# A linear-attention and mixture kernel on one core: receptances and state as fp16 pairs, and the low part of the values on GpSimd

## The reference

```python
# stage 1, for 4 batches and 8 heads, 768 tokens, 48 dims a head
for t in range(S):
    cur = einsum('bhd,bhe->bhde', u * k[t], v[t])
    y[t] = einsum('bhd,bhde->bhe', r[t], state + cur)
    state = w[t][:, None] * state + einsum('bhd,bhe->bhde', k[t], v[t])
x = y as (3072 tokens, 384)
# stage 2
h = x @ w_in;  g = h * clip(h + 3, 0, 6) / 6;  x = g @ w_out
# stage 3: soft mixture of 8 experts with 4 slots each
logits = x @ phi; softmax over tokens fills 32 slots, each expert applies
w1, relu, w2 to its slots; softmax over slots gives each token its output
```

## Time and profile before

| | before |
|---|---|
| median of 3 runs | 421.21 us (420.39 to 424.60) |
| span of the profiled execution | 418.7 us |
| PE busy | 402.8 us, 96% |
| DVE busy | 338.7 us, 81% |
| POOL busy | 187.7 us, 45% |
| ACT busy | 162.3 us, 39% |
| granted TensorE clock, mean | 0.992 |

### The profile page before, as it was taken

One profiled execution on the slowest core, in us unless ns is written; L12 is line 12 of the kernel. 1 busy time (PEld: TensorE's weight loads), 2 busy tenths in 40 slices (PEclk: granted clock), 3 DMA queues, 4 the chain that ended last, 5 costly groups with the idle time before them and its releaser, 6 DMA issues.

```text
span 418.7 us, 9789 instructions
## 1 busy us (share of the span) xinstructions
PE 402.8 (96%) x3913; PEld 220.6 (53%) x3913; DVE 338.7 (81%) x561; ACT 162.3 (39%) x299; POOL 187.7 (45%) x178
## 2 busy tenths in 40 slices
PE   8999999999999999999999999999999999999981
PEld 3885555555555555555555555455453444544430
DVE  7998799998998888989989998989975787662152
ACT  3586255533343244144433433351333234321141
POOL 4445988865465655445743556464450012010000
PEclk9999999999999999999999999999999999999996
DMA  8997321468043123314430331331006189869929
GB/s 250 358 398 274 123 83 43 124 237 291 21 124 123 55 71 125 97 29 124 125 112 13 122 102 36 112 122 59 0 4 261 43 347 419 257 254 415 407 106 358
DMA packets 16541, 69.35 MB, mean 166 GB/s; under 512 B 2160, under 2 KB 3184, under 8 KB 14832
## 3 DMA queue, kind: packets, MB, share of 16 engines
q1 hardware_dynamic: 16496, 68.73, 46.9%
HBM read 64.00 MB, written 4.72 MB: 164 GB/s over the span
## 4 chain that ended last, share of the span: by engine, by line
issue 36%; PE 26%; POOL 22%; DVE 7%; DMA 5%; ACT 1%; POOLq 0%; SPq 0%; DVEq 0%
POOL att L1552 5%; DMA att<-rkT_dram 4%; POOL att L1514 4%; PE hid L578 4%; POOL att L1516 4%; PE hid L580 4%; PE hid L579 4%; POOL att L1537 3%; POOL att L1570 3%; POOL w_split L1528 3%; PE hid L846 3%; PE hid L827 1%; PE sc_ps L827 1%; DVE gated L1009 1%; PE l_ps L626 1%
## 5 line engine op out<-in xcount | busy, mean ns | idle before, releaser
L1361 ACT ACTIVATE relu<-hid,three 128x512 f32<-128x512 f32 x95 | 65.1, 686 | 136.5 <-PE hid L580 136.2
L578 PE MATMUL hid<-x_split,w_split 128*128 128x512 f16 x285 | 108.3, 380 | 0.5 <-DVE gated L1009 0.4
L580 PE MATMUL hid<-x_split,w_split 128*128 128x512 f16 x285 | 108.0, 379 | 0.0
L579 PE MATMUL hid<-x_split,w_split 128*128 128x512 f16 x285 | 108.0, 379 | 0.0
L1009 DVE SCALAR_TENSOR_TENSOR gated<-relu,hid 128x512 f32<-128x512 f32 x95 | 64.3, 677 | 22.0 <-ACT relu L1361 21.3
L1030 DVE STREAM_TRANSPOSE ring<-gated 128x512 f32<-128x512 f32 x96 | 68.3, 711 | 3.3
L1543 POOL TENSOR_TENSOR att<-att 128x1024 f16<-128x1024 f32 x20 | 40.9, 2046 | 49.1 <-ACT att L1296 49.1
L1561 POOL TENSOR_TENSOR att<-att 112x512 f32<-112x512 f32 x19 | 23.2, 1222 | 55.8 <-DVE att L928 55.8
L578 PEld LDWEIGHTS hid<-x_split,w_split 128*128 128x128 f16 x285 | 27.7, 97 | 37.3 <-DVE gated L1009 6.8
L580 PEld LDWEIGHTS hid<-x_split,w_split 128*128 128x128 f16 x285 | 27.8, 98 | 33.7
L579 PEld LDWEIGHTS hid<-x_split,w_split 128*128 128x128 f16 x285 | 27.9, 98 | 24.9 <-issue 0.3
(11 more groups left out here) (276 smaller groups left out, 759.6 us busy)
## 6 DMA issues: line engine op xcount, KB each, us to landing
att<-nat_dram SPq DMA_DIRECT2D x20, 576.0 KB, 4.2
att<-rkT_dram SPq DMA_DIRECT2D x22, 448.0 KB, 5.6
att<-wT_dram SPq DMA_DIRECT2D x22, 226.2 KB, 4.8
att<-w_dram SPq DMA_DIRECT2D x3, 1536.0 KB, 9.7
out_dram<-w_split SPq DMA_DIRECT2D x11, 384.0 KB, 3.9
att<-w_dram SPq DMA_DIRECT2D x5, 768.0 KB, 10.7
stage<-w_in_dram SPq DMA_DIRECT2D x2, 1536.0 KB, 13.2
ring<-w_outT_dram SPq DMA_DIRECT2D x1, 3072.0 KB, 15.2
```

Source lines behind the costliest of these rows:

```text
L578: pe.matmul(hid[s % 2][:], high, x_high, start=(q == 0), stop=False)
L579: pe.matmul(hid[s % 2][:], high, x_low, start=False, stop=False)
L580: last = pe.matmul(hid[s % 2][:], low, x_high, start=False, stop=(q == KT - 1))
L1361: nc.scalar.activation(relu_tile(s), hid[s % 2][:], ACT.Relu, bias=three[:], scale=GATE / H_SCALE)\
```

## The change

- The roles of the two scans are exchanged. `scan_prefix` runs first, over `mark`, and gives the product of the decays from the chunk's **first** token on (times `R_SCALE` = 256); `restart_suffix` takes the reciprocal of the whole product and `scan_suffix` runs second. ACT's new `save_decay` copies the chunk's product to a small tile.
- Receptances and state go into `attend` as fp16 pairs. ACT rounds (`high_receptance`, 112 x 512; `high_state`, 112 x 384), POOL subtracts (`low_receptance`, `low_state`). In `attend` three fp16 matmuls of 96 columns stand for the fp32 one. The fp32 receptances have one buffer instead of two, so the decay of unit n+1's waits for unit n's `score`.
- `decay_state(n)` now comes after unit n's increment has been added, and is done two phases of other units ahead of its use, with `high_state` and `low_state` behind it.
- Values: ACT scales them in place, then rounds the scaled ones (two ACT instructions instead of one); POOL subtracts. DVE's `low_v` is gone. The scales of `copy_keys`, `high_x` and `finish_y` are adapted.
- In the first four units POOL decays the receptances and DVE the keys (before: the other way round).

```diff
             def attend(n):
                 b = n % B
                 pe.wait_ge(x_lo_done, n)
-                pe.wait_ge(decayed, n - B + 1)
+                pe.wait_ge(state_lo_done, n - B + 1)
+                pe.wait_ge(r_lo_done, n - B + 1)
                 pe.wait_ge(v_lo_done, n - B + 1)
                 pe.wait_ge(scores_lo_done, n - B + 1)
...
-                    pe.matmul(both, r_dec[n % 2][0:PD, p * P:(p + 1) * P], state[b][0:PD, p, :],
-                              start=True, stop=False, skip_group_check=True)
+                    pe.matmul(both, r_hi[0:PD, tokens], state_hi[b][0:PD, p, :], start=True, stop=False,
+                    pe.matmul(both, r_hi[0:PD, tokens], state_lo[b][0:PD, p, :], start=False, stop=False,
+                    pe.matmul(both, r_lo[0:PD, tokens], state_hi[b][0:PD, p, :], start=False, stop=False,
...
-            def low_v(n):
-                dve.wait_ge(v_hi_done, n - B + 1)
-                nc.vector.scalar_tensor_tensor(v_lo[n % 2], nat_of(n, 2), V_SCALE, v_hi[n % 2],
-                                               ALU.mult, ALU.subtract).then_inc(v_lo_done, 1)
...
-                nc.scalar.activation(v_hi[n % 2], nat_of(n, 2), ACT.Copy, scale=V_SCALE).then_inc(v_hi_done, 1)
+                nc.scalar.activation(nat_of(n, 2), nat_of(n, 2), ACT.Copy, scale=V_SCALE).then_inc(v_scaled, 1)
+                act.wait_ge(v_scaled, n - B + 1)
+                nc.scalar.activation(v_hi[n % 2], nat_of(n, 2), ACT.Copy).then_inc(v_hi_done, 1)
...
+            def save_decay(n):
+                act.wait_ge(prefix_done, n + 1)
...
+            def high_receptance(n):
+                act.wait_ge(r_dec_done, n + 1)
+                if n > B:
+                    act.wait_ge(y_ready, n)
+                nc.scalar.activation(r_hi[0:PD], r_dec[0:PD], ACT.Copy).then_inc(r_hi_done, 1)
+
+            def high_state(n):
+                act.wait_ge(decayed, n + 1)
+                if n >= B:
+                    act.wait_ge(y_ready, n + 1)
+                nc.scalar.activation(state_hi[n % B][0:PD], state[n % B][0:PD], ACT.Copy).then_inc(state_hi_done, 1)
...
+            def low_v(n):
+                pool.wait_ge(v_hi_done, n - B + 1)
+                nc.gpsimd.tensor_tensor(v_lo[n % 2], nat_of(n, 2), v_hi[n % 2], ALU.subtract).then_inc(v_lo_done, 1)
...
             def decay_receptance(n):
                 pool.wait_ge(prefix_done, n + 1)
                 pool.wait_ge(rk_rows_in[n % B], 16 * (n // B + 1))
-                if n >= 2:
-                    pool.wait_ge(scores_ready, 2 * (n - 1))
-                    pool.wait_ge(y_ready, n - 1)
+                pool.wait_ge(scores_ready, 2 * n)
+                if n > B:
+                    pool.wait_ge(r_lo_done, n - B)
...
+            def low_receptance(n):
+                pool.wait_ge(r_hi_done, n - B + 1)
+                nc.gpsimd.tensor_tensor(r_lo[0:PD], r_dec[0:PD], r_hi[0:PD], ALU.subtract).then_inc(r_lo_done, 1)
...
+            def low_state(n):
+                pool.wait_ge(state_hi_done, n + 1)
+                nc.gpsimd.tensor_tensor(state_lo[n % B][0:PD], state[n % B][0:PD], state_hi[n % B][0:PD], ALU.subtract)\
+                    .then_inc(state_lo_done, 1)
```

More of the change, by code:

```diff
@@ L116, in build_program @@
         last_max = stats[:, 7:8]
+        chunk_decay = [stats[:, i:i + PB] for i in (32, 36, 64, 68)]
+        state_hi, state_lo = ([pairs(spare[:, first + b * PB * D:first + (b + 1) * PB * D].bitcast(F16), 2 * D) for b in range(B)]
+                              for first in (2 * PB, 2 * PB + B * PB * D))
         w_early = {2: gated[:, 0:SCAN], 3: relu[:, 0:SCAN]}
@@ L479, in score @@
                         rows = slice(ALIGN * j, ALIGN * j + D)
-                        last = pe.matmul(sc_bank[j][:, cols], k_dec[n % 2][rows, cols], r_dec[n % 2][rows, cols],
+                        last = pe.matmul(sc_bank[j][:, cols], k_dec[n % 2][rows, cols], r_dec[rows, cols],
                                          start=True, stop=True)
```

160 lines of the change are left out of this document (101 added, 59 removed).

## The result

| | before | changed |
|---|---|---|
| median | 420.80 us (4 runs, 420.20 to 424.60) | 425.89 us (4 runs, 425.04 to 426.11) |
| span of the profiled execution | 418.7 us | 424.3 us |
| granted TensorE clock, mean | 0.992 | 0.976 |
| attend(4), attend(7), attend(8), attend(23) start | 42.54, 82.42, 95.57, 311.63 | 48.10, 95.62, 108.49, 317.19 |

The ratio to the kernel before is 1.011, with a 95% interval of 1.007 to 1.015: slower by about 1%.

A forecast was written before the change was run, and what follows sets the result against it. POOL was taken to bound the kernel as much as PE up to 82 us, PE from unit 8 on. 6.0 + 6.9 - 8.4 = +4.5 on 418.7 gives 423.2, plus 2.5 to the median: 425.7 us, range 415.5 to 432.

The forecast's parts named there:

- Term 1: Up to attend(4): POOL's added work, a delayed start and collisions with DVE make attend(4) later, +6.0 us (2.5 to 7.5).
- the two collisions: Ahead of attend(4): unit 5's second scan and DVE's low_w each hold up POOL, adding 1.6 us.
- Term 2: Units 5 to 7: POOL's work and collisions set the pace, 46.8 us in place of 39.9, +6.9 (1.5 to 8.4).
- follow each other: DVE instructions with two SBUF inputs and POOL instructions take turns; each collision costs POOL about 0.9 us.
- Term 3: From attend(7) on: attends save 0.62 us each, 10.5 in all, less 2.1 for POOL: -8.4 us (-10.5 to -3).
- POOL in a light unit: Units without weight pieces: 7.87 us, 3.1 of added subtractions and two collisions of 0.9 make 12.8 us.
- the early stretch keeps PE's pace: Rival, up to unit 7: POOL's additions fit, nothing is lost, 12.4 us saved, 408.8 us; chance 0.24.
- POOL sets the light units' pace: Rival, light units: they stay at 13.0 to 13.1 us, sum +9.9, 431.1 us; chance 0.17.
- The clock fell as feared: Rival, PE's waits before attend(4) and the next three: clock returns at 0.50, +2 to +4 us, 428.7; chance 0.09.

The follow-up runs named there:

- e4: Against the kernel before: only the new order of decays, saved decay column and ScalarE's value scaling; attend in fp32, low values on DVE. 421.16 us, ratio 1.001.
- e6: Changed kernel plus 20 fp16 matmuls of 512 columns that keep PE busy ahead of attend(4)'s wait. 432.74 us, ratio 1.030.
- e9: Changed kernel with POOL waiting for the first scan in units 5, 6 and 7, ahead of its weight pieces. 426.51 us, ratio 1.012.
- e2: Changed kernel, but units 4 to 7 attend in fp32 with two receptance tiles and low values on DVE; pairs from unit 8 on. 413.77 us, ratio 0.983.
- e3: Changed kernel with the low values moved from POOL back to DVE, without the scales that go with it. 437.06 us, ratio 1.039.
- e10: Changed kernel with both the POOL waits of e9 and the PE-warming matmuls of e6. 426.05 us, ratio 1.011.
- e1: Changed kernel with one added wait: in unit 6 POOL waits for the first scan ahead of its weight pieces. 423.2 us, ratio 1.008.

## Why the prediction came out, step by step

The total is nearer than its parts, and by luck. The terms give +4.5 and the span moved by 5.6. What closes the gap between 425.7 and 425.9 is the 2.5 us added for the distance from the profiled span to the median, which is 1.6 in the changed kernel (424.3 and 425.9).

- **Term 1, attend(4): +6.0 predicted, +5.6 measured.** It waits for POOL's `low_scores`, and the two collisions are there as assumed (`low_state` at 39.48 took 1.79, `low_scores` 2.72):

```profile
45.24 2.72 POOL L1596 TENSOR_TENSOR att<-att 128x1024 f16<-128x1024 f32 x1
...
48.10 0.24 PE L560 MATMUL y_ps<-spare,att 112*128 112x96 f16 x1 [4.75 <-POOL att L1596]
```

  Of it the order of the decays has 0.9 (e4), the pairs and the low values the rest. The three POOL subtractions are a little cheaper than assumed, 1.09, 0.87 and 0.87 us in place of 1.2, 1.0 and 1.0 (the medians of L1618, L1583 and L1632).
- **Term 2, units 5 to 7: +6.9 predicted, +7.6 measured, and here the mechanism was only half right.** Predicted were 14.8, 16.0 and 16.0 us, measured 14.0, 19.4 and 14.1. The failing step is that DVE and POOL "follow each other": in an unbroken run of POOL instructions a scan can lose every boundary. That also changed the path. attend(5) and attend(7) started 0.26 and 0.25 us behind the end of POOL's `low_v`, as predicted; attend(6) started 4.1 us behind it (`low_v` ended at 77.46), held up by the gate behind the starved scan and by matmuls at a granted clock of 0.50. POOL took 13.9 us from the end of `low_scores(4)` to that of `low_v(5)`, then 15.6 and 17.9 from one `low_v` to the next. In the first of these there was no collision, where I had counted two, but a wait of 1.22 for ACT. The second is the predicted case. The third has one collision and a wait of 3.19 for the second scan, which the starved one had made late:

```profile
81.78 1.18 POOL L1605 TENSOR_TENSOR att<-att 112x512 f32<-112x512 f32 x1 [3.19 <-DVE att L950]
```

  Errors of opposite sign met; the sum is better than its mechanism. e6 shows how little it takes for the same code to lose 7 us more.
- **Term 3, behind attend(7): -8.4 predicted, -7.6 measured.** An attend saves 0.52 us, not 0.62. I had multiplied the second head pair's 0.44 by four; the first pair takes 211.24 to 211.59 = 0.35. The price of the fp16 matmuls, 0.04 each, was right:

```profile
207.47 0.21 PE L560 MATMUL y_ps<-spare,att 112*128 112x96 f16 x1
207.52 0.20 PE L562 MATMUL y_ps<-spare,att 112*128 112x96 f16 x1
207.56 0.20 PE L564 MATMUL y_ps<-spare,att 112*128 112x96 f16 x1
```

  17 times 0.52 is 8.8, and 1.2 went elsewhere, where I had taken off 2.1 for POOL. But 1.05 of the 1.2 has nothing to do with what I had in mind. A DVE instruction of stage 3's running sum, 128 x 1, stood in front of POOL's `decay_receptance` in this execution and took 1.27 us, where it takes 0.22 in e9:

```profile
288.26 1.27 DVE L1100 SCALAR_TENSOR_TENSOR stats<-stats 128x1 f32<-128x1 f32 x1
...
288.33 1.19 POOL L1614 TENSOR_TENSOR att<-att 112x512 f32<-112x512 f32 x1
```

```profile
289.39 0.22 DVE L1100 SCALAR_TENSOR_TENSOR stats<-stats 128x1 f32<-128x1 f32 x1
```

  From attend(20) to attend(22) the changed kernel took 29.62 us and e9 28.57. Whether it happens in the executions that were not profiled is not known. POOL in a light unit was put at 12.8 and is 11.04: one collision at most, not two.
- **The rivals.** That the early stretch keeps PE's pace was refuted by the trace, and e2 shows the kernel for which it holds. That POOL sets the light units' pace did not happen, but e3 shows that it was near: 0.6 to 1.0 us more on DVE, in the loop of the two engines, and the gain is gone. The clock fell as feared (0.50 between 46 and 52 us, before and behind attend(4), as in the window above), but its price behind attend(4) is lost in the spread (e9 and e10). PE stood still less than I had said: 4.75 us before attend(4) in place of 7, and 0.56 at most before each of the next three in place of 3.5.
- **What stays open:** the exact condition of the starved scan, as said, the 128 x 1 instruction that does not fit it, and e1's long executions.

## What to carry to other kernels

Where an engine has room in most of a kernel but not in one stretch, apply the change only where the room is: from attend(8) on the changed kernel gains 7.4 us, and its pairs, with the low values on POOL, cost 10.8 ahead of it (against e2). A sum of busy times does not show a loop of two engines that wait for each other; undo the companion part of a change by itself to see whether the loop fits. And before a run of GpSimd instructions is made unbroken beside VectorE instructions with two SBUF inputs, look at the longest of these, not at their mean.

## What was not expected of the hardware

- A VectorE scan of 1.2 us took up to 7.3 beside GpSimd in the kernels and 8.1 in a kernel of its own, there 28 times of 28 where it started in a 112-partition instruction of an unbroken run, and never in 20 where it started ahead of it. That the partitions are the cause was only argued.
- A small gain upstream (a scan that began 1 us earlier, with the clock kept at 1.00) cost 7 us downstream: three scans then started in such a place.
- A copy of 512 fp32 columns from SBUF to SBUF on VectorE waits for GpSimd like an instruction with two SBUF inputs (up to 2.47 us); a product with one input in PSUM does not (0.68 in each of six).
- A VectorE instruction on 128 x 1 values took 1.27 us in place of 0.22 beside a GpSimd instruction of 1.19 us, and the kernel's attends came 1.05 later for it.
